# Attention and two feed-forward layers on one core: the first load split over two queues, one warm-up product fewer

## The reference

```python
# attention: batch 4, heads 8, seq 768, head_dim 64; chunk 32, 16 left, 8 right, 8 memory keys
for c in range(nc):
    k_full = concat([mem_k, k_ctx]); v_full = concat([mem_v, v_ctx])      # 64 keys per chunk
    scores = scale * matmul(q_c, k_full.T); scores -= max(scores)
    a = exp(scores); a = a / (sum(a) + 1e-9)
    out[c] = matmul(a, v_full)
# first layer: 3072 tokens, 512 -> 1024 -> 512
h = x @ w_in; sm = softmax(h); solu = h * sm; ln = normalise(solu) * g_ln; x = ln @ w_out
# second layer: 512 -> 2048 -> 512
h = x @ w_in; g = maximum(0.01 * h, h); out = g @ w_out
```

## Time and profile before

| | us |
|---|---|
| median of 3 runs | 803.44 |
| lowest, highest | 802.81, 803.88 |
| the profiled execution's own time | 801.41 |
| its span | 799.6 |

### The profile page before, as it was taken

How to read it: one execution, slowest core, us unless ns; L and a number is a source line. 1 busy time by engine, 2 the same in 40 slices (tenths; PEclk the granted TensorE clock), 3 DMA queues, 4 the chain that set the end, 5 groups by cost and what they waited for, 6 DMA issues and landing times.

```text
span 799.6 us, 14400 instructions
## 1 busy us (share of the span) xinstructions
PE 792.2 (99%) x5582; PEld 650.3 (81%) x5582; DVE 541.4 (68%) x902; ACT 453.8 (57%) x737; POOL 62.6 (8%) x156
## 2 busy tenths in 40 slices
PE   8999999999999999999999999999999999999998
PEld 5888888888888888888888888888888888888886
DVE  7988889987532656247452335666799698779775
ACT  4768887777443356255464447666645555545543
POOL 1233333322100000000000000000000000000000
PEclk9999999999999999999999999999999999999999
DMA  9956876865848875176774577545923740462002
GB/s 358 334 178 208 279 221 230 234 165 161 283 89 287 319 252 185 52 245 226 248 255 158 211 247 240 178 172 173 386 115 101 271 146 26 148 249 104 27 1 79
DMA packets 79892, 156.72 MB, mean 196 GB/s; under 512 B 6225, under 2 KB 30929, under 8 KB 79825
## 3 DMA queue, kind: packets, MB, share of 16 engines
q1 hardware_dynamic: 79824, 155.81, 57.7%
HBM read 99.16 MB, written 56.62 MB: 195 GB/s over the span
## 4 chain that ended last, share of the span: by engine, by line
PE 98%; DVE 1%; issue 0%; ACT 0%; POOL 0%; ACTq 0%
PE hid_a L732 24%; PE hid_b L732 24%; PE scores_ps L732 22%; PE attn_ps L732 14%; PE probs_ps L732 7%; PE attn_ps L724 3%; PE scores_ps L698 2%; PE probs_ps L710 1%; PE hid_b L846 0%; DVE unit_max L1164 0%; DVE shifted L1167 0%; DVE unit_sum L1176 0%; DVE w_in_lo L1146 0%; ACT prob L867 0%; POOL prob L1427 0%
## 5 line engine op out<-in xcount | busy, mean ns | idle before, releaser
L861 ACT ACTIVATE ring_hi<-g_blk 128x512 fp32r<-128x512 f32 x168 | 105.9, 632 | 108.1 <-PE hid_b L732 40.4
L1146 DVE TENSOR_TENSOR ring_lo<-g_blk,ring_hi 128x512 fp32r<-128x512 f32 x168 | 115.6, 688 | 38.6 <-ACT ring_hi L861 35.5
L1010 ACT ACTIVATE g_out<-g_out 128x512 f32<-128x512 f32 x72 | 45.4, 630 | 71.7 <-DVE g_out L1272 41.5
L732 PE MATMUL scores_ps<-x_op_P_hi,w_hi 128*128 128x512 f32 x144 | 56.1, 390 | 0.0
L732 PE MATMUL scores_ps<-x_op_P_lo,w_hi 128*128 128x512 f32 x144 | 56.0, 389 | 0.0
L732 PE MATMUL scores_ps<-x_op_P_hi,w_lo 128*128 128x512 f32 x144 | 56.0, 389 | 0.0
L732 PE MATMUL hid_b<-ring_hi,w_hi 128*128 128x512 f32 x128 | 49.9, 390 | 0.0
L732 PE MATMUL hid_b<-ring_lo,w_hi 128*128 128x512 f32 x128 | 49.8, 389 | 0.0
L732 PE MATMUL hid_b<-ring_hi,w_lo 128*128 128x512 f32 x128 | 49.8, 389 | 0.0
L1146 DVE TENSOR_TENSOR x_op_P_lo<-op_raw,x_op_P_hi 128x1024 fp32r<-128x1024 f32 x21 | 25.7, 1224 | 20.4 <-ACT x_op_P_hi L861 20.3
L732 PE MATMUL hid_a<-w_in_hi,xT_hi 128*128 128x512 f32 x96 | 39.4, 410 | 0.0
(11 more groups left out here) (178 smaller groups left out, 2041.0 us busy)
## 6 DMA issues: line engine op xcount, KB each, us to landing
g_scratch<-g_out SPq DMA_DIRECT2D x96, 256.0 KB, 2.6
g_blk<-g_scratch SPq DMA_DIRECT2D x48, 512.0 KB, 7.7
attn_buf<-qk_in SPq DMA_DIRECT2D x32, 576.0 KB, 6.6
attn_buf<-v_in SPq DMA_DIRECT2D x32, 384.0 KB, 4.3
ln_scratch<-lnT SPq DMA_DIRECT2D x24, 512.0 KB, 6.2
w_raw<-w_in SPq DMA_DIRECT2D x16, 512.0 KB, 4.1
ln_even<-ln_scratch SPq DMA_DIRECT2D x12, 512.0 KB, 6.7
ln_odd<-ln_scratch SPq DMA_DIRECT2D x12, 512.0 KB, 6.6
```

The costliest lines, as they stand in the source:

```text
L732: mm = pe.matmul(psum, weights[i], data[j], start=first and n == 0, stop=last and n == 2, skip_group_check=goes_on)
L861: return act.activation(dst, src, ACT.Copy)
L1010: act.activation(x, x, ACT.Prelu, alpha=0.01).then_inc(s_g[q], 1)
L1146: return ve.tensor_tensor(dst, x, hi.bitcast(f32), ALU.subtract)
```

## The change

Two edits. The first product step of `START` issues two wide products in place of three. And the load of unit 0's queries and keys is issued as two DMAs: partitions 0 to 63 by SyncE as before, partitions 64 to 127 by ScalarE as the first instruction of its program, with a semaphore of its own, `s_qk_first`, for which `scores(0)` waits as well (it multiplies both halves). `ROWS` is 64. All other loads are as they were.

```diff
 START = (
-        ("keep_warm", 3, 288), ("load_qk", 0), ("load_qk", 1), ...
+        ("keep_warm", 2, 288), ("load_qk", 0), ("load_qk", 1), ...

+        s_qk_first = sem("s_qk_first")

             def load_qk(a):
                 if a >= SLOTS:
                     sp.wait_ge(s_scores, a - SLOTS + 1)
-                sp.dma_start(attn_buf[a % SLOTS][:, 0:BLOCK + SEG], qk_in[a]).then_inc(s_qk_in[a % SLOTS], 16)
+                rows = slice(0, ROWS if a == 0 else P)
+                sp.dma_start(attn_buf[a % SLOTS][rows, 0:BLOCK + SEG], qk_in[a, rows]).then_inc(s_qk_in[a % SLOTS], 16)

             def scores(a):
                 slot = a % SLOTS
                 pe.wait_ge(s_qk_in[slot], 16 * (a // SLOTS + 1))
+                if a == 0:
+                    pe.wait_ge(s_qk_first, 16)

         @block.scalar
         def _(act):
+            act.dma_start(attn_buf[0][ROWS:, 0:BLOCK + SEG], qk_in[0, ROWS:]).then_inc(s_qk_first, 16)
```

More of the change, by code:

```diff
@@ L110 @@
 START = (
-        ("keep_warm", 3, 288), ("load_qk", 0), ("load_qk", 1), ("load_ident",), ("load_w1", 0), ("load_v", 0),
+        ("keep_warm", 2, 288), ("load_qk", 0), ("load_qk", 1), ("load_ident",), ("load_w1", 0), ("load_v", 0),
         ("load_qk", 2), ("load_qk", 3), ("load_w1", 1),
```

## The result

The changed kernel takes 805.88 us (median of 6 runs, 805.55 to 806.73), the kernel before, run beside it, 803.31 (801.59 to 803.88): a ratio of 1.0031 with a 95% interval of 1.0019 to 1.0043. It is slower by 2.6 us, above the 0.2% line and outside the stated range. The profiled execution has a span of 803.8 us and an own time of 805.63, so its span is 4.2 us longer than that of the profile before. Part of that is a matter of which execution was profiled, as will be seen.

The account below looks back on a forecast made before the run. TensorE, busy 792.2 of 799.6 us, was taken as the bound, with its last wait ending at 17.55 us. Removed product, ScalarE's issue, added wait and unit 0's landing each counted 0, giving 803.4 us; range 802.4 to 804.6.

Parts of the forecast that it names:

- The first product step: Before `scores(0)`: one product fewer takes 1.08 us off TensorE's warm work but becomes a 0.9 us wait; worth 0.
- the 17.55: Start in us of `probs_t` of unit 2, where TensorE's last wait ends; the forecast asked only whether the change moves it.
- Rival C: TensorE's clock stays low longer after the hole before `scores(0)`: 804.3, chance 0.08; lasting through 12 to 18 us: 808, chance 0.04.
- From there to the end nothing holds TensorE up.: After `probs_t` of unit 2 starts at 17.55 us TensorE never waits, so nothing there can swallow or repay a shift.
- When does unit 0 land: Landing of unit 0's split load: no change or 0.1 us early, bounded by 0.8 us earlier and 1.5 us late.
- rival B: ScalarE's half of unit 0 comes last, 1.5 us late, less 0.4: +1.1, 804.5; chance 0.08.
- Rival E: Each half of unit 0 is served at half the rate, landing up to 0.7 us later: +0.3, 803.7; chance 0.08.
- The cost is d - 0.4.: If `scores(0)` is later by d, `shift(3)` on VectorE is too, and 0.40 us of idle behind it absorbs part.
- the weight piece: Weight piece 1, whose split `w1_hi(1)` on ScalarE was to begin still at 14.10 us, when the piece lands.
- ScalarE's issue: One more DMA before ScalarE's table load, moving it back by at most 1.28 us, hidden in 4.95 us of idle: 0.
- an earlier unit 0: Unit 0 landing up to 0.1 us earlier: worth 0 by way of ScalarE, at most 0.22 us on TensorE's side.
- Rival A: Two queues shorten the DMA ramp, every later load lands earlier, 17.55 moves by at most 0.8 us: 802.6; chance 0.12.

Follow-up runs that it names:

- thin loads: Against the changed kernel: for units 4 to 7 only the first eighth of the columns of queries, keys and values is loaded; 803.73 us.

## Why the prediction was wrong

**"The first product step ... it becomes a wait of about 0.9 us for the DMA. Cover of this edit at nothing."** The arithmetic was right (0.78 us of idle, `scores(0)` at 4.50), and so nearly was the step as far as the prediction followed it: alone, the missing product moved the 17.55 by 0.2 us. The price was not: it costs a ratio of 1.0022, 2.5 us between the medians, and the kernels without a hole (four products, or five with the split) do not pay it. The product was what kept TensorE busy until the clock rose, and the prediction put that at nothing outside a rival. Rival C named this low clock, with 0.9 us and 8 in 100. Its first steps came out as worked (2.50 for 2.4, 0.97 for 0.97) and the third shorter (2.14 for 2.9), but its way to a loss, a later `shift(3)` and 0.9 us at `probs_t` of unit 2, did not occur: 0.2 us arrived there. What it lacked was what stands behind, the wait for instructions and the second fall of the clock.

**"From there to the end nothing holds TensorE up."** This is the step that failed. In the changed kernel a wait of 1.86 us stands behind that point, then one of 0.37 at 38.1 us. The earlier trace rows are true of that execution and not of the kernel. The prediction noted that the profiled own time of 801.41 lay 2.0 us under the median of 803.44, and used it as an offset. It was a symptom: 801.41 lies under the lowest of the three runs shown, so the profile was probably of an execution that lacked something which the timed ones had. Another execution of the same kernel, of 803.17 us, has a wait of 1.89 us that ends at 21.4; the one of 801.51 has none. This step made every rival too cheap.

**"When does unit 0 land": "no change or 0.1 us early".** This term was wrong too. Unit 0 landed 1.5 us late, at the upper end of the bounds, by another way than rival B: it was SyncE's half that came last. Rival E's mechanism is what the runs show: the Trainium skill's *SBUF — State Buffer*, "Door 1: The DMA port swizzle", says that partitions 0 to 63 reach half of the ports, and 64 to 127 the other half, and 221 GB/s in place of 402 to 411, on one queue as on two, and 413 once each half spans all 128 partitions, agree. I had given it 0.7 us by letting the other loads fill the gaps; they did not: between 4 and 5 us all queues together moved 221 GB/s, unit 1 among it. The Trainium skill's *DMA: Bandwidth & Descriptors*, "Rules for kernel authors", advises against two transfers to disjoint partition halves because they serialize; the q10 row (nothing on SyncE's queue until 3 us) agrees, though from 3 to 4 us both queues moved data.

**"The cost is d - 0.4."** With d = 1.5 this gives 1.1; `probs_t` of unit 2 came 1.5 later. Near in size, but not by the way that was worked out: the weight piece, taken as fixed at 14.10, itself landed 1.1 us later, and TensorE went into `probs_t` of unit 2 without a wait, straight from `values` of unit 1.

**Right**: ScalarE's issue and its shifted table load cost nothing (ScalarE waited 5.81 us before its first exponential), and the removed product could not bring in its 1.08 us. That an earlier unit 0 would be worth nothing is not shown: no run had it earlier by more than 0.1 us, and the split by columns with three products (0.9998) had `scores(0)` 0.2 us later. Rival A did not occur: the stream moved later, not earlier.

What stays open is why a low clock between 5 and 10 us goes with late instructions ten microseconds later. It is not lateness alone: four and five products came later and had no wait, or 0.20, and the missing product with the load whole had TensorE only 0.2 us late when it ran out of instructions. That the instructions wait among the data in the DMA engines is supported by the thin loads (1.86 to 0.79), not shown in full. One run does not fit the hole as the whole price: two products with the shorter third step have hole, slow step and wait, and yet a ratio of 1.0008 (0.9992 to 1.0024), an interval that leaves room for both. Nor is it traced why two executions of one kernel differ in when the clock rises.

## What to carry to other kernels

Before costing a change, compare the profiled execution's own time with the runs: if it lies outside them, its list of waits may not be the kernel's, and a second profile is worth more than a finer reading of the first. Filler work in front of a wait is part of the schedule: take it out only if what it covers gets shorter by as much, and be wary of a stretch in which TensorE has not yet reached its upper clock. A point up to which a delay is absorbed is not the end of its account: here 0.2 us arrived there and 2.5 us were lost. To share a load over two queues, cut it so that each part spans all partitions; two such loads on two queues were served evenly, whichever was wanted first.

## What the runs showed of the hardware

- Loads of 64 partitions (0 to 63, then 64 to 127) ran at 221 GB/s with the DMA share at 1.03 to 1.05; the same bytes over 128 partitions at 413.
- Two DMAs of 576 KB issued at 0.72 us on two queues landed after 5.3 and 5.4 us; the first of two on one queue had landed after 3.8.
- With a hole of 0.78 us in TensorE's first 5 us the following step took 2.50 us in place of 1.64. A stretch with 1.50 of 3.50 us busy was followed by 3.4 us at the lower clock in one profile; after a longer wait, 2.41 us, the clock did not fall.
- TensorE can stand for 1.9 us and more between two equal instructions with nothing to wait for but its own instructions: behind its 345th matmul record in 9 of 16 profiles, and for 0.79 and 0.20 us in two more. Each time it went on 2.3 to 2.6 us after the start of a 16 KB packet on q8.
